# An RWKV attention in doubling blocks: r kept packed, its spread form copied by ScalarE

## The chip, the cores and the metric

One core of one Trainium2 chip. The time is the device time of one launch in microseconds; what is compared is the median of several runs. The engines are TensorE (PE in the profile; PEld is its weight load), VectorE (DVE), ScalarE (ACT), GpSimd (POOL) and SyncE (SP), which here only issues transfers.

## What is computed

Three stages in fp32: a recurrent attention with a decaying state per batch and head (4 batches, 8 heads, 768 tokens, 48 channels a head), a gated layer with RMS norm (384 to 1536 to 384), and a layer that takes the largest of three products (384 to 768 to 384).

```python
for t in range(S):
    kt, vt, rt, wt = (k[:, :, t], v[:, :, t], r[:, :, t], w[:, :, t])
    cur = np.einsum('bhd,bhe->bhde', u[None] * kt, vt)
    y[:, :, t] = np.einsum('bhd,bhde->bhe', rt, state + cur)
    state = wt[:, :, :, None] * state + np.einsum('bhd,bhe->bhde', kt, vt)
...
xn = x / rms * rms_g; g = xn @ w_gate
x1 = (silu(g) * (xn @ w_val)) @ w_out
...
out = maximum(maximum(x1 @ w1, x1 @ w2), x1 @ w3) @ w_out2
```

## The kernel before

The tokens are cut into six tiles of 128. In a tile the attention runs two batches ("a duo", j = 0 and 1) at a time. Channels lie on the partitions, two heads side by side: rows 0 to 63 hold the even head of a pair, rows 64 to 127 the odd one, and four pairs lie along the free axis. The recurrence is solved by doubling: at level L, blocks of h = 2^L tokens are joined in pairs. There are seven levels, 0 to 6. At each level and for each j:

- TensorE (`scores`, L477, levels 1 to 6) multiplies k with the right halves of r. Its moving operand needs r *spread*: `rB[j]` has a plane for the even heads, zero in the odd heads' rows, and one for the odd heads, zero in the others, so that one product of 128 rows yields the scores of each head by itself. Eight matmul records stand for one group of four matmuls.
- VectorE (`rescale_r_even`, L877) multiplies the right halves of r by the decay of the left block, in the even heads' rows, 64 rows of 256 columns; GpSimd (`rescale`, L1119 and L1124) multiplies the left halves of k (128 rows) and then the odd heads' r (64 rows). Both work on rB in place; at the last level they write to the packed `rD[j]`, whose left halves ScalarE copies from rB (`copy_r_left`, L682).
- VectorE takes the scores into A under a mask (`take_scores`, L900; a plain copy, L906, at level 6) and multiplies the block decays together (`double_blocks`, L887), which waits for r and k of the step.

After level 6, TensorE brings k back to tokens first (L511), computes the attended values from rD and the state (L495), and updates the state (L518).

**Slots.** Each engine has the same program of 18 slots a duo: slot 2L + j follows step j of level L, and four more come at the end (`TAIL_AT` = 14). A slot holds a part of the gated layer of the tile before: of each three parts, one is the gate product (TensorE L459 to L461, then ScalarE's sigmoid L672), one the value product (then VectorE's two products L853 and L856), one the output product (ScalarE's high part h_hi L676, GpSimd's low part h_lo L1091). Each engine goes through its own list strictly in this order.

**Tile 0** is different. In its first duo there is no gated layer yet; slots 3, 5, 7, 9, 11, 13 and 14 hold the splitting of one weight piece each: ScalarE writes the high part (`weight_piece`, L661), then VectorE the low part (L841, L843). In its second duo (`second_duo_slot`) a slot holds two parts of the layer, on half of the tokens (the batches of the first duo), and in slots 0 to 10 a weight piece behind them. ScalarE issues a piece's load two pieces ahead. Tile 1 also has half-sized parts (the other batches), without weights; from tile 2 on (a loop, `Fori`) the parts have full size. After the last tile come the last parts and the third stage, with three loops of its own.

**Queues.** SyncE issues the loads of k and w (`load_kw`), the tokens, r (`load_r`, two transfers of 128 KB, one per head row half) and v in the order written. At the start it waits until VectorE has zeroed rB before it loads r. ScalarE's queue issues the weight loads.

Of the kernel before, what the change touches and what calls it, by code (L numbers as in the profile page):

```python
# [45 lines left out]
def rwkv_moe_kernel(nc, rc, kc, wc, r, k, v, u, g_w1, v_w1, o_w1, rms_g, w1, w2, w3, o_w2, out):  # L46
# [17 lines left out]
    with ExitStack() as ctx:  # L64
# [34 lines left out]
        rD = [at_(f"rD{j}", [P, PAIRS, T]) for j in range(2)]  # L99
# [71 lines left out]
        r_even_scaled = sem("r_even_scaled")  # L171
        r_odd_scaled = sem("r_odd_scaled")
        r_left_copied = sem("r_left_copied")
# [65 lines left out]

        def r_rights(j, level, o):  # L240

            rows, h = HEAD_ROWS[o], 1 << level
            old = half(rB[j][rows, o, :, :], h, 1)
            return (half(rD[j][rows, :, :], h, 1) if level == LEVELS - 1 else old), old
# [94 lines left out]
        def _(sp):  # L339
# [114 lines left out]
        def _(pe):  # L454
# [8 lines left out]
            def scores(a, duo, level, j):  # L463
# [4 lines left out]
                after(pe, r_even_scaled, a, STEPS, n - 1)  # L468
                after(pe, r_odd_scaled, a, STEPS, n - 1)
# [10 lines left out]
            def attended(a, duo, j):  # L480
# [8 lines left out]
                after(pe, r_even_scaled, a, STEPS, n + 1)  # L489
                after(pe, r_odd_scaled, a, STEPS, n + 1)  # L490
                after(pe, r_left_copied, a, 2 * B, 2 * b + 2)
                after(pe, scores_used, a, SCORES, score(duo, LEVELS - 1, j) + 1)
                after(pe, v_in[j], a, 16 * DUOS, 16 * (duo + 1))
                for q in range(PAIRS):
                    mm(ps_desk[:, q * 2 * D:(q + 1) * 2 * D], rD[j][:, q, :], state[:, b * PAIRS + q, :],  # L495
                       start=(q == 0), stop=False)
# [150 lines left out]
        def _(act):  # L647
# [183 lines left out]
        def _(dve):  # L831
# [33 lines left out]
            def rescale_r_even(a, duo, level, j):  # L865

                n = step(duo, level, j)
# [358 lines left out]
```

## Time and profile before

| | |
|---|---|
| time, median of 3 runs | 1063.11 us (1062.24 to 1064.55) |
| span of the profiled execution | 1055.6 us |
| TensorE | 1010.7 us busy, 96% of the span |
| VectorE | 630.4 us, 60% |
| GpSimd | 493.3 us, 47% |
| ScalarE | 251.6 us, 24% |
| L1119 k product on GpSimd | 168 times, 142.9 us |
| L1124 odd r product on GpSimd, into rB | 144 times, 120.0 us (and 24 times into rD) |
| L877 even r product on VectorE, into rB | 144 times, 96.5 us (and 24 times into rD) |

The span is what the profiler sees from the first to the last instruction; the time of a run holds a little more around it. A busy share is an average over stages with different limits: what a change is worth has to be read in the stage where it acts, by looking at which engine's wait ends last there.

### The profile page before, as it was taken

Reading aid. Unit: us, or ns where it says so; the run is one execution under the profiler, and the core shown is the slowest. Engines: PE = TensorE matmul, PEld = TensorE weight load, DVE = VectorE, ACT = ScalarE, POOL = GpSimd, SP = SyncE. Lnnn points to the kernel's source line nnn. Section 1 sums busy time; section 2 is a strip of 40 time slices with the busy share of each in tenths; the row PEclk is TensorE's granted clock in tenths of the full one; section 3 lists DMA queues with packets and bytes.
Section 4 is the critical chain, followed back from the end, with each engine's and each line's share of the span. In section 5 each row is a group of like instructions: output and inputs, shape, how many; then the busy total and the mean of one; then the engine's idle time right before and its main releaser. Section 6 shows DMA issues by size and latency. Waiting matters only on the chain.

```text
span 1055.6 us, 17238 instructions
## 1 busy us (share of the span) xinstructions
PE 1010.7 (96%) x5760; PEld 884.7 (84%) x5760; DVE 630.4 (60%) x1083; ACT 251.6 (24%) x500; POOL 493.3 (47%) x548
## 2 busy tenths in 40 slices
PE   4778989899999999999999999999999999999998
PEld 4678988888888888888888888888788888888887
DVE  8978798987776877687787777444331312121221
ACT  1233312222122121312122212323331212121211
POOL 7655586767574756565756757121020201011111
PEclk9789999999999999999999999999999999999999
DMA  6533212303111221204030310211301010101000
GB/s 198 161 94 105 77 54 68 93 30 117 34 65 57 85 65 43 76 1 137 11 108 12 117 33 4 90 45 47 118 1 60 1 60 9 51 15 45 22 7 30
DMA packets 36216, 64.56 MB, mean 61 GB/s; under 512 B 4928, under 2 KB 22720, under 8 KB 36160
## 3 DMA queue, kind: packets, MB, share of 16 engines
q1 hardware_dynamic: 30288, 52.12, 15.4%
q10 hardware_dynamic: 5872, 11.80, 3.8%
q8 instruction: 23, 0.38, 0.1%
q14 instruction: 33, 0.27, 0.1%
HBM read 54.46 MB, written 9.44 MB: 61 GB/s over the span
## 4 chain that ended last, share of the span: by engine, by line
PE 84%; DVE 6%; POOL 5%; issue 3%; ACT 1%; DMA 0%; SPq 0%; POOLq 0%; DVEq 0%
PE ps_sc L477 9%; PE ps_acc L459 8%; PE ps_acc L461 8%; PE ps_acc L460 8%; PE ps_gate L459 6%; PE ps_val L459 5%; PE ps_val L461 5%; PE ps_gate L460 5%; PE ps_gate L461 5%; PE ps_val L460 5%; PE ps_desk L500 4%; PE ps_sc L460 2%; PE ps_sc L459 2%; PE ps_sc L461 2%; POOL kT L1119 2%
## 5 line engine op out<-in xcount | busy, mean ns | idle before, releaser
L477 PE MATMUL ps_sc<-rB,kT 128*128 128x128 f32 x1152 | 161.5, 287 | 25.8 <-DVE A L900 12.4
L477 PEld LDWEIGHTS ps_sc<-rB,kT 128*128 128x128 f32 x1152 | 154.9, 200 | 37.2 <-DVE rB L877 19.6
L1119 POOL TENSOR_TENSOR kT<-kT,wT 128x256 f32<-128x256 f32 x168 | 142.9, 851 | 86.0 <-PE ps_sc L477 58.1
L1184 POOL TENSOR_TENSOR h_lo<-h2f,h_hi 128x512 fp32r<-128x512 f32 x36 | 46.4, 1290 | 253.6 <-ACT h_hi L822 253.6
L1091 POOL TENSOR_TENSOR h_lo<-act_h,h_hi 128x512 fp32r<-128x512 f32 (+1 forms) x83 | 98.1, 1182 | 109.5 <-ACT h_hi L676 104.4
L1124 POOL TENSOR_TENSOR rB<-rB,wT 64x256 f32<-64x256 f32 x144 | 120.0, 833 | 11.3
L877 DVE TENSOR_TENSOR rB<-rB,wT 64x256 f32<-64x256 f32 x144 | 96.5, 675 | 37.8 <-PE ps_sc L477 28.4
L459 PE MATMUL ps_gate<-x_hi,wg_hi 128*128 128x512 f32 (+1 forms) x252 | 97.4, 386 | 7.7 <-DVE act_h L853 5.8
L676 ACT ACTIVATE h_hi<-act_h 128x512 fp32r<-128x512 f32 (+1 forms) x84 | 48.0, 571 | 227.9 <-DVE act_h L856 227.6
L900 DVE COPY_PREDICATED A<-mask,ps_sc 128x512 f32<-128x512 uint8 x120 | 98.7, 822 | 0.0
L672 ACT ACTIVATE act_h<-ps_gate 128x512 f32<-128x512 f32 (+1 forms) x84 | 45.0, 536 | 217.7 <-PE ps_gate L461 217.6
L459 PE MATMUL ps_val<-x_hi,wv_hi 128*128 128x512 f32 (+1 forms) x252 | 96.6, 383 | 0.0
L459 PE MATMUL ps_acc<-h_hi,wo_hi 128*128 128x512 f32 (+1 forms) x252 | 95.8, 380 | 0.5 <-POOL h_lo L1091 0.3
L461 PE MATMUL ps_val<-x_hi,wv_lo 128*128 128x512 f32 (+1 forms) x252 | 92.0, 365 | 0.0
L460 PE MATMUL ps_val<-x_lo,wv_hi 128*128 128x512 f32 (+1 forms) x252 | 91.8, 364 | 0.0
L460 PE MATMUL ps_gate<-x_lo,wg_hi 128*128 128x512 f32 (+1 forms) x252 | 91.5, 363 | 0.0
L461 PE MATMUL ps_gate<-x_hi,wg_lo 128*128 128x512 f32 (+1 forms) x252 | 91.4, 363 | 0.0
L461 PE MATMUL ps_acc<-h_hi,wo_lo 128*128 128x512 f32 (+1 forms) x252 | 90.9, 361 | 0.0
L460 PE MATMUL ps_acc<-h_lo,wo_hi 128*128 128x512 f32 (+1 forms) x252 | 90.8, 360 | 0.0
L1067 DVE TENSOR_TENSOR h2f<-h2f,ps_val 128x512 f32<-128x512 f32 x18 | 12.4, 688 | 108.1 <-PE ps_val L461 108.1
L887 DVE TENSOR_TENSOR wT<-wT 128x256 f32<-128x256 f32 (+6 forms) x168 | 65.1, 399 | 17.6 <-POOL rB L1124 16.1
L856 DVE TENSOR_TENSOR act_h<-act_h,ps_val 128x512 f32<-128x512 f32 (+1 forms) x84 | 51.4, 612 | 40.1 <-PE ps_val L461 38.9
(135 smaller groups left out, 2071.8 us busy)
## 6 DMA issues: line engine op xcount, KB each, us to landing
kT<-in_k_channels SPq DMA_DIRECT2D x24, 256.0 KB, 3.5
wT<-in_w_channels SPq DMA_DIRECT2D x24, 256.0 KB, 4.0
rB<-in_r_channels SPq DMA_DIRECT2D x48, 128.0 KB, 2.7
kL<-in_k_tokens SPq DMA_DIRECT2D x24, 192.0 KB, 2.4
rL<-in_r_tokens SPq DMA_DIRECT2D x24, 192.0 KB, 2.5
vL<-in_v_tokens SPq DMA_DIRECT2D x24, 192.0 KB, 2.4
x_scratch<-x1s SPq DMA_DIRECT2D x6, 768.0 KB, 4.3
xn<-x_scratch SPq DMA_DIRECT2D x6, 768.0 KB, 4.3
```

The costliest lines, as they stand in the source:

```text
L459: mm(dst, lhs[0], rhs[0], start=start, stop=False)
L460: mm(dst, lhs[0], rhs[1], start=False, stop=False)
L461: return mm(dst, lhs[1], rhs[0], start=False, stop=stop)
L477: last = mm(ps_sc[:, j, q * T:(q + 1) * T], kT[2 * duo + j][:, q, :], rights, start=True, stop=True)
L676: nc.scalar.activation(h_hi[:, f % 2, toks], act_h[:, f % 2, toks], ACT.Copy).then_inc(h_hi_done, 1)
L856: tt(hidden, hidden, ps_val[:, toks], ALU.mult).then_inc(val_used, 1)
L877: tt(new, old, block_decay(2 * duo + j, 1 << level, 0, HEAD_ROWS[0]), ALU.mult).then_inc(r_even_scaled, 1)
L887: tt(left, left, half(w[:, :, :], h, 1)[:, :, 0:1], ALU.mult).then_inc(tot_done, 1)
L900: nc.vector.copy_predicated(dst, every_head.broadcast_to([P, H, n, h]), src.rearrange("p (g n h) -> p g n h", g=H, h=h)).then_inc(scores_u ...
L1091: tt(h_lo[:, f % 2, toks], act_h[:, f % 2, toks], h_hi[:, f % 2, toks].bitcast(F32), ALU.subtract).then_inc(h_lo_done, 1)
L1119: tt(half(kT[b][:, :, :], h, 0), half(kT[b][:, :, :], h, 0), block_decay(b, h, 1), ALU.mult).then_inc(k_scaled, 1)
L1124: tt(new, old, block_decay(b, h, 0, HEAD_ROWS[1]), ALU.mult).then_inc(r_odd_scaled, 1)
```

## The change

r is loaded, scaled and used in the packed form `rP[j]` (rows as in k). One product on VectorE per level and j scales all 128 rows. GpSimd only scales k. ScalarE copies the right halves for the next level into rB, two copies of 64 rows (`spread_r`), and no longer copies left halves. The copies of level L + 1 stand in ScalarE's list at step j of level L, ahead of the slot, and wait for VectorE's product of that step. TensorE's scores wait for the copies. `load_r` becomes one transfer without a wait; the wait for the zeroed rB moves to ScalarE's first copy.

```diff
             def load_r(b, a):
-                for o, rows in enumerate(HEAD_ROWS):
-                    sp.dma_start(rB[b % 2][rows, o, :, :], rc[b, a, o]).then_inc(r_in[b % 2], 16)
+                sp.dma_start(rP[b % 2][:, :, :], rc[b, a].rearrange("o d q t -> (o d) q t")).then_inc(r_in[b % 2], 16)
...
                 load_kw(b, 0)
-                if b == 0:
-                    sp.wait_ge(rb_zeroed, 2)
                 load_r(b, 0)
...
             def scores(a, duo, level, j):
-                after(pe, r_even_scaled, a, STEPS, n - 1)
-                after(pe, r_odd_scaled, a, STEPS, n - 1)
+                after(pe, r_spread, a, 2 * SCORES, 2 * score(duo, level, j) + 2)
                 after(pe, k_scaled, a, STEPS, n - 1)
...
             def attended(a, duo, j):
-                after(pe, r_even_scaled, a, STEPS, n + 1)
-                after(pe, r_odd_scaled, a, STEPS, n + 1)
-                after(pe, r_left_copied, a, 2 * B, 2 * b + 2)
+                after(pe, r_scaled, a, STEPS, n + 1)
...
-            def copy_r_left(a, duo, j):
-                after(act, scores_done, a, SCORES, score(duo, LEVELS - 1, j) + 1)
-                for o, rows in enumerate(HEAD_ROWS):
-                    nc.scalar.activation(rD[j][rows, :, 0:T // 2], rB[j][rows, o, :, 0:T // 2], ACT.Copy
-                                         ).then_inc(r_left_copied, 1)
+            def spread_r(a, duo, level, j):
+                h = 1 << level
+                if isinstance(a, int) and a == duo == 0 and level == 1:
+                    act.wait_ge(rb_zeroed, j + 1)
+                after(act, scores_done, a, SCORES, score(duo, level, j) - 1)
+                after(act, r_scaled, a, STEPS, step(duo, level - 1, j) + 1)
+                for o, rows in enumerate(HEAD_ROWS):
+                    nc.scalar.activation(half(rB[j][rows, o, :, :], h, 1), half(rP[j][rows, :, :], h, 1), ACT.Copy
+                                         ).then_inc(r_spread, 1)
...
                     for j in range(2):
-                        if level == LEVELS - 1:
-                            copy_r_left(a, duo, j)
+                        if level < LEVELS - 1:
+                            spread_r(a, duo, level + 1, j)
                         slot(2 * level + j)
...
-            def rescale_r_even(a, duo, level, j):
+            def rescale_r(a, duo, level, j):
+                n, h = step(duo, level, j), 1 << level
                 if level:
                     after(dve, tot_done, a, STEPS, n - 1)
-                    after(dve, r_even_scaled, a, STEPS, n - 1)
+                    after(dve, r_scaled, a, STEPS, n - 1)
+                    after(dve, r_spread, a, 2 * SCORES, 2 * score(duo, level, j) + 2)
+                    after(dve, scores_done, a, SCORES, score(duo, level, j) + 1)
...
-                new, old = r_rights(j, level, 0)
-                tt(new, old, block_decay(2 * duo + j, 1 << level, 0, HEAD_ROWS[0]), ALU.mult).then_inc(r_even_scaled, 1)
+                rights = half(rP[j][:, :, :], h, 1)
+                tt(rights, rights, block_decay(2 * duo + j, h, 0), ALU.mult).then_inc(r_scaled, 1)
...
             def double_blocks(a, duo, level, j):
-                after(dve, r_even_scaled, a, STEPS, n + 1)
-                after(dve, r_odd_scaled, a, STEPS, n + 1)
+                after(dve, r_scaled, a, STEPS, n + 1)
                 after(dve, k_scaled, a, STEPS, n + 1)
...
-            def rescale(a, duo, level, j):
+            def rescale_k(a, duo, level, j):
-                after(pool, k_scaled, a, STEPS, n + 1)
-                new, old = r_rights(j, level, 1)
-                tt(new, old, block_decay(b, h, 0, HEAD_ROWS[1]), ALU.mult).then_inc(r_odd_scaled, 1)
-                after(pool, r_odd_scaled, a, STEPS, n + 1)
```

## Rows read from the trace of the kernel before

**Rows 1.** Busy time by stretch: start:end, length, PE, PEld, DVE, ACT, POOL, clock, DMA

```profile
0.00:50.00 50.00, 29.25 (x152) 26.71 (x152) 42.92 (x67) 11.50 (x18) 36.24 (x54) 0.86 0.60 182
50.00:106.00 56.00, 44.98 (x333) 42.91 (x333) 46.36 (x79) 17.39 (x35) 31.16 (x33) 0.91 0.34 100
106.00:217.00 111.00, 101.77 (x860) 98.64 (x859) 96.94 (x189) 28.23 (x75) 77.99 (x97) 1.00 0.24 74
220.00:664.00 444.00, 444.00 (x2622) 387.20 (x2620) 337.94 (x606) 100.80 (x205) 282.98 (x314) 1.00 0.18 57
```

**Rows 2.** What TensorE waited for, 50 to 106 us, then 106 to 217: us, times, longest

```profile
PE ps_gate L459 <- DVE act_h L853: 5.8, 6, 1.8
...
PE ps_sc L477 <- DVE A L900: 5.3, 4, 1.8
```

**Rows 3.** What VectorE waited for, 0 to 50 us, then 106 to 217

```profile
DVE wT L887 <- POOL rB L1124: 1.7, 1, 1.7
...
DVE wT L887 <- POOL rB L1124: 3.3, 5, 1.1
```

**Rows 4.** Two lines over the whole span: ns min/median/max, first and last start

```profile
L877 DVE TENSOR_TENSOR rB<-rB,wT x144: 406/452/1430, 7.9 to 648.4; 64x256 f32<-64x256 f32 x144
...
L682 ACT ACTIVATE rD<-rB x48: 402/417/421, 38.3 to 654.0; 64x256 f32<-64x256 f32 x48
```

**Rows 5.** VectorE by line and shape from 7, 50, 106 and 217 us: busy, mean ns

```profile
L877 DVE TENSOR_TENSOR rB<-rB,wT 64x256 f32<-64x256 f32 x12 | 7.4, 613 | 1.5 <-DMA rB<-in_r_channels 1.3 <-PE ps_sc L477 0.2
...
L877 DVE TENSOR_TENSOR rB<-rB,wT 64x256 f32<-64x256 f32 x12 | 9.3, 777 | 0.0
L887 DVE TENSOR_TENSOR wT<-wT 128x32 f32<-128x32 f32 x2 | 0.9, 430 | 0.0
...
L877 DVE TENSOR_TENSOR rB<-rB,wT 64x256 f32<-64x256 f32 x24 | 16.6, 697 | 0.1
...
L887 DVE TENSOR_TENSOR wT<-wT 128x32 f32<-128x32 f32 x16 | 3.3, 205 | 0.0
```

**Rows 6.** GpSimd's L1124 from 50 to 106 us, grouped; then two in order of time

```profile
L1124 POOL TENSOR_TENSOR rB<-rB,wT 64x256 f32<-64x256 f32 x12 | 12.3, 1025 | 0.9
...
69.90 1.65 DVE L843 SCALAR_TENSOR_TENSOR wg_lo<-x1s,gcol,wg_hi 128x768 fp32r<-128x768 f32 x1 [1.32 <-ACT wg_hi L661]
...
70.82 1.45 POOL L1124 TENSOR_TENSOR rB<-rB,wT 64x256 f32<-64x256 f32 x1
```

**Rows 7.** ScalarE, then VectorE, in order of time, 74.7 to 78 us

```profile
74.71 0.42 ACT L676 ACTIVATE h_hi<-act_h 128x256 fp32r<-128x256 f32 x1 [3.75 <-DVE act_h L856]
75.61 0.38 ACT L672 ACTIVATE act_h<-ps_gate 128x256 f32<-128x256 f32 x1 [0.48 <-PE ps_gate L461]
...
75.89 0.93 ACT L661 ACTIVATE wg_hi<-xn,gcol 128x768 fp32r<-128x768 f32 x1
...
76.41 0.96 DVE L877 TENSOR_TENSOR rB<-rB,wT 64x256 f32<-64x256 f32 x1
77.31 0.71 DVE L900 COPY_PREDICATED A<-mask,ps_sc 128x512 f32<-128x512 uint8 x1
77.92 1.52 DVE L843 SCALAR_TENSOR_TENSOR wg_lo<-xn,gcol,wg_hi 128x768 fp32r<-128x768 f32 x1
```

**Rows 8.** VectorE, then ScalarE, where the second half of tile 0 begins

```profile
55.77 0.42 DVE L877 TENSOR_TENSOR rB<-rB,wT 64x256 f32<-64x256 f32 x1
...
55.89 0.38 ACT L706 ACTIVATE x_hi<-ps_gate 128x256 fp32r<-128x256 f32 x1 [2.43 <-PE ps_gate L533]
```

**Rows 9.** ScalarE, then VectorE, at the start

```profile
12.00 0.20 ACT L775 ACTIVATE warm<-gcol 128x1 f32<-128x1 f32 x1 [1.00 <-DMA ub<-in_u]
...
13.63 1.06 DVE L877 TENSOR_TENSOR rB<-rB,wT 64x256 f32<-64x256 f32 x1
```

**Rows 10.** ScalarE, then TensorE, after the loop's top

```profile
335.16 0.60 ACT L672 ACTIVATE act_h<-ps_gate 128x512 f32<-128x512 f32 x1 [0.61 <-PE ps_gate L461]
...
336.99 1.98 PE L477 MATMUL ps_sc<-rB,kT 128*128 128x128 f32 x16
```

More of the change, by code:

```diff
@@ L98, in rwkv_moe_kernel @@
         rB = [at_(f"rB{j}", [P, 2, PAIRS, T]) for j in range(2)]
-        rD = [at_(f"rD{j}", [P, PAIRS, T]) for j in range(2)]
+        rP = [at_(f"rP{j}", [P, PAIRS, T]) for j in range(2)]
         kT = [at_(f"kT{b}", [P, PAIRS, T]) for b in range(B)]
@@ L170, in rwkv_moe_kernel @@
         u_taken = sem("u_taken")
-        r_even_scaled = sem("r_even_scaled")
-        r_odd_scaled = sem("r_odd_scaled")
-        r_left_copied = sem("r_left_copied")
+        r_scaled = sem("r_scaled")
+        r_spread = sem("r_spread")
         k_scaled = sem("k_scaled")
@@ L238, in block_decay @@
             return c.broadcast_to([rows.stop - rows.start, PAIRS * T // (2 * h), h])
[L240 to L244, printed above, removed]
         MASKED = LEVELS - 2
@@ L863, in last_hidden_lo @@
                    ).then_inc(last_h_lo, 1)
-            def rescale_r_even(a, duo, level, j):
-                n = step(duo, level, j)
+            def rescale_r(a, duo, level, j):
+                n, h = step(duo, level, j), 1 << level
                 if level:
                     after(dve, tot_done, a, STEPS, n - 1)
-                    after(dve, r_even_scaled, a, STEPS, n - 1)
+                    after(dve, r_scaled, a, STEPS, n - 1)
+                    after(dve, r_spread, a, 2 * SCORES, 2 * score(duo, level, j) + 2)
+                    after(dve, scores_done, a, SCORES, score(duo, level, j) + 1)
                 else:
                     after(dve, kw_in[2 * duo + j], a, 32, 32)
-                    after(dve, r_in[j], a, 32 * DUOS, 32 * (duo + 1))
-                if level:
-                    after(dve, scores_done, a, SCORES, score(duo, level, j) + 1)
-                new, old = r_rights(j, level, 0)
-                tt(new, old, block_decay(2 * duo + j, 1 << level, 0, HEAD_ROWS[0]), ALU.mult).then_inc(r_even_scaled, 1)
+                    after(dve, r_in[j], a, 16 * DUOS, 16 * (duo + 1))
+                rights = half(rP[j][:, :, :], h, 1)
+                tt(rights, rights, block_decay(2 * duo + j, h, 0), ALU.mult).then_inc(r_scaled, 1)
             def double_blocks(a, duo, level, j):
                 n, h = step(duo, level, j), 1 << level
-                after(dve, r_even_scaled, a, STEPS, n + 1)
-                after(dve, r_odd_scaled, a, STEPS, n + 1)
+                after(dve, r_scaled, a, STEPS, n + 1)
                 after(dve, k_scaled, a, STEPS, n + 1)
@@ L997, in duo_steps @@
                 for level in range(LEVELS):
-                    rescale_r_even(a, duo, level, 0)
+                    rescale_r(a, duo, level, 0)
                     take_scores(a, duo, level, 0)
                     slot(2 * level)
-                    rescale_r_even(a, duo, level, 1)
+                    rescale_r(a, duo, level, 1)
                     take_scores(a, duo, level, 1)
@@ L1111, in rescale @@
                     after(pool, tot_done, a, STEPS, n - 1)
-                    after(pool, r_odd_scaled, a, STEPS, n - 1)
                     after(pool, k_scaled, a, STEPS, n - 1)
+                    after(pool, scores_done, a, SCORES, score(duo, level, j) + 1)
                 else:
                     after(pool, kw_in[b], a, 32, 32)
-                    after(pool, r_in[j], a, 32 * DUOS, 32 * (duo + 1))
-                if level:
-                    after(pool, scores_done, a, SCORES, score(duo, level, j) + 1)
-                tt(half(kT[b][:, :, :], h, 0), half(kT[b][:, :, :], h, 0), block_decay(b, h, 1), ALU.mult
-                   ).then_inc(k_scaled, 1)
-                after(pool, k_scaled, a, STEPS, n + 1)
-                new, old = r_rights(j, level, 1)
-                tt(new, old, block_decay(b, h, 0, HEAD_ROWS[1]), ALU.mult).then_inc(r_odd_scaled, 1)
-                after(pool, r_odd_scaled, a, STEPS, n + 1)
+                lefts = half(kT[b][:, :, :], h, 0)
+                tt(lefts, lefts, block_decay(b, h, 1), ALU.mult).then_inc(k_scaled, 1)
             def inverse_rms(a, duo, j):
@@ L1135, in duo_steps @@
                     for j in range(2):
-                        rescale(a, duo, level, j)
+                        rescale_k(a, duo, level, j)
                         slot(2 * level + j)
```

2 lines of the change are left out of this document (1 added, 1 removed).

## The prediction

> **What bounds the kernel now.** I read the busy time by stretch first. From 220 to 664 us TensorE is busy for 444.00 of 444 us at full clock, so nothing done to the other engines can shorten that part, as long as they don't become late [rows 1]. In the first 217 us it idles: 20.8 us up to 50, 11.0 us from 50 to 106, 9.2 us from 106 to 217. Everything after 664 us is code that the change doesn't touch. So the whole case lies in tile 0 (up to about 106 us) and in the attention of tile 1 (up to 217 us).
>
> Next, who makes TensorE wait there. It is VectorE: its gate product L853 for 5.8 us, then its taking of scores L900 for 5.3 us [rows 2]. VectorE itself hardly idles (46.4 us busy of 56, 96.9 of 111 [rows 1]) and loses time on GpSimd in two ways. It waits outright for the odd heads' r, 1.7 and 3.3 us [rows 3]. And its operations stretch when a GpSimd operation runs beside them: the r product needs 0.406 us undisturbed [rows 4] but 0.613, 0.777 and 0.697 us on average in the three stretches; the small wT product of level 3 takes 0.430 us there against 0.205 us later [rows 5]. An L843 of 1.65 us lies across an L1124 of 1.45 us: each is held up by the other [rows 6].
>
> **The change, part by part.** The sum goes by differences; the profiled span is 1055.6 us, 7.5 us under the median of 1063.11 us, and I keep these 7.5 us. A difference of 0.2%, 2.1 us, is about what a measurement of this kernel can tell from none.
>
> *VectorE's r product* covers 128 rows instead of 64. The wT product of the same 256 columns on 128 rows runs at the same rate, so I cost this at nothing; the bound from the other side is none either, since the count stays 168.
>
> *GpSimd loses 168 products.* In 50 to 106 us they are 12.3 of its 31.2 us, 39% [rows 1, 6]. What VectorE gets back there: L877 loses 12 x (0.777 - 0.406) = 4.5 us, L887 about 12 x (0.430 - 0.205) = 2.7 us (one level's excess taken for all), and I add 1 us for the weight operations, so 8 us, of which 39% is 3.1 us. One more us for k's products, which meet a VectorE that now idles more. Before 50 us: 12 x (0.613 - 0.406) = 2.5, 14 x 0.225 = 3.1, another 0.5, so 6 us; 39% is 2.4 us, with the 1.7 us of plain waiting 4.1 us. From 106 to 217: 24 x (0.697 - 0.406) = 7.0 and 28 x 0.225 = 6.3 us, so 13 us; its 28 products are a smaller part of GpSimd's 78.0 us, and I take 30%: 3.9 us, with the 3.3 us of waiting 7.2 us.
>
> That two operations stretch rather than share is what the Trainium skill says too (SBUF — State Buffer, section "SBUF: two separate sides"): the port pair of VectorE and GpSimd is an exclusive lock, and the loser blocks for the whole instruction. By it a removed GpSimd operation may free more than its share of time, since each block moves the next one; that is rival A.
>
> *ScalarE gets 288 copies of 64x256 and loses 48.* The copies that it has take 0.417 us [rows 4], so 240 x 0.417 = 100 us on an engine with 251.6 us of work in 1055.6. Its load costs nothing; its order does. The two copies stand ahead of each slot's other work and wait for VectorE's product of the same step, so all that ScalarE had done early now comes after it. Who waits for that:
>
> - In tile 0's second half VectorE's low-part operation of each slot needs ScalarE's high part. In the slots with h_hi and the next sigmoid (1, 4, 7, 10), ScalarE does h_hi, sigmoid and high part from 74.71 to 76.8 us, before VectorE begins the step at 76.41; VectorE finds them done [rows 7]. Now they follow the r product: 0.83 + 0.42 + 0.28 + 0.93 = 2.46 us, of which VectorE's taking of scores covers 0.61 (77.31 to 77.92). New wait 1.85 us, three times, and 2.0 us in slot 1, which takes no scores: 7.5 us. In two slots with sigmoid first, VectorE's gate product waits 1.21 - 0.7 = 0.5 us: 1.0 us. In the slots where h_hi waits for VectorE anyway, nothing.
> - At this half's start ScalarE's x_hi at 55.89 falls behind copies that wait for the product of 55.77 + 0.42 [rows 8]: 56.19 + 0.83 = 57.0, so 1.1 us.
> - In the first half the high part follows the copies: 0.83 + 0.93 = 1.76 us, of which 0.8 is covered. 0.95 us at four levels, 0.4 at level 1, whose taking of scores is longer: 4.2 us. For new meetings with k's product I add 0.4 us.
> - At the start the first copy waits until ScalarE is through with its constants at 12.2 us [rows 9]. SyncE now issues r in one transfer, without waiting for the zeroing of rB, and reaches u's transfer nearly 3 us sooner, so I expect the copy at 10 to 12.2 us and the second r product of VectorE (13.63 us) between 13.1 and 15 us. Taken as 0; bounds -0.5 and +1.6.
> - In the tiles from 2 on the copies lie in slack, since a score group comes 5 us after the product that feeds it. The tightest place is the loop's top: ScalarE's sigmoid at 335.16, scores at 336.99 in two groups of 0.9 us [rows 10]. Copies at 335.2 to 336.0 and, after the sigmoid, 336.6 to 337.45 are 0.4 us early for the second group at 337.9. So 0; if the copy at level 1, with runs of two elements, takes twice 0.417, it is 1 us late at each of the four tops: bounds 0 and +4.
>
> *The wait that replaces the odd heads' one* on TensorE, for the copies instead of two scalings, is met 0.9 us after VectorE's product, where the taking of scores that it already waits for ends after 0.7 us. In tile 1 that lies within the slack of some 1.4 us per group.
>
> *Tile 1's attention* (106 to 217) has no weight pieces, so only relief: 7.2 us for VectorE against 9.2 us of TensorE idle. What is late next is TensorE itself, and the two levels where VectorE works on the neighbour terms (some 0.8 us left per half, and 0.9 us at the end). I take 6.5 us; bounds 4 and 9.
>
> *Sum.* First half of tile 0: -4.1 + 4.2 + 0.4 + 0 = +0.5. Second half: -4.1 + 7.5 + 1.0 + 1.1 = +5.5. Tile 1: -6.5. Later: 0. Together -0.5 us: 1055.1 us of span, 1062.6 us of time. That is no change.
>
> **The rivals.** A, the lock gives back more: all of VectorE's excess in tile 0 goes (14 us instead of the 6.5 us counted), as far as products can be freed of it. Then -7.5 more, less some 2 us where TensorE becomes the bound: -6, 1057 us. For it: blocks chain in rows 6. Against it: k's product starts on the same signal as r's and stays. Chance 0.34.
>
> B, slower: ScalarE's order in tile 0. Place: the weight slots; price: 1.85 us at three or four slots and 0.95 at five, which also thin TensorE's work, and its clock averages 0.86 and 0.91 there already [rows 1]. It decides from the point where tile 0 loses more than tile 1's 6.5 us and the 2.1 us of a visible change, 8.6 us. If the relief in tile 0 comes to half (4 us instead of 8.2), tile 0 loses 10 us, and with 1 to 3 us of low clock the sum is +5 to +7: 1069 us. Chance 0.22.
>
> C, the late copy at the loop's tops, +4 on top of the forecast: 1066 us. Chance 0.06. That the change does not do what it says cannot be: the products leave GpSimd's program.
>
> **How the numbers follow.** The forecast's case, the two effects cancelling within 2.1 us, has 0.38. Faster by over 0.2% is A and a fringe: 0.36. Slower is B and C: 0.28. Same: 0.36. The range takes in A's 1057 and B's 1069: 1056.5 to 1069.
>
> **What would show it.** Right: VectorE's L877 successor near 0.45 us on average and no wait of VectorE for GpSimd's r; new waits of VectorE for ScalarE's weight operation, 1.8 us each, in slots 1, 4, 7, 10 and 1 us at levels 1 to 5; tile 1's TensorE idle down to 2 or 3 us; no idle after 220 us. Wrong: weight waits absent (then A), TensorE idle in tile 1 still over 5 us (then B), idle at each loop top (C).

## The result, and the profile after

The changed kernel takes 1071.3 us (1069.93 to 1072.36) against 1062.67 us of the kernel before beside it: 1.0085 times, 95% interval 1.0062 to 1.0107. Executed again, beside other executions of the kernel before, it took 1068.7 us, 1.0059 times (1.0042 to 1.0076). It is slower by 6 to 9 us; the forecast was 0.5 us faster, with 1069.0 as the upper end.

First the page's engine line and the granted clock in 40 slices of the changed kernel, then its busy time by stretch (start:end, length, PE, PEld, DVE, ACT, POOL, clock, DMA share, GB/s).

```profile
PE 1016.3 (95%) x5760; PEld 889.0 (83%) x5760; DVE 619.7 (58%) x1083; ACT 351.4 (33%) x740; POOL 348.5 (33%) x380
...
PEclk9679999999999999999999999999999999999999
```

```profile
0.00:50.00 50.00, 24.45 (x124) 22.25 (x124) 36.36 (x61) 18.82 (x35) 21.40 (x39) 0.79 0.54 177
50.00:106.00 56.00, 44.38 (x302) 42.20 (x302) 34.56 (x65) 22.42 (x49) 12.93 (x18) 0.83 0.26 77
106.00:217.00 111.00, 101.49 (x843) 98.38 (x843) 96.18 (x194) 45.96 (x115) 52.79 (x65) 0.98 0.27 80
```

The work moved as planned: GpSimd went from 493 to 349 us busy, ScalarE from 252 to 351. Against [rows 1] VectorE is busy for 12 us less between 50 and 106 us, and TensorE still gets less done there (302 matmuls, not 333), at a lower clock. Half of the 12 us is work that now lies behind 106 us: for the same work, between the first two marks of the next table, VectorE is busy for 53.7 us where before's second trace has 59.7.

To see where time goes I take four marks in TensorE's program: its first transposition of x (L520; L533 before) in tile 0's second half, at the start and at the end of tile 1's attention, and the last one, at the end of tile 5. In the trace of before they stand at 55.2, 126.7, 215.1 and 671.9 us. So the second half of tile 0 lasts to 126.7 us on TensorE; the prediction ended it at 106, with its last scores, but TensorE waits for nothing between 106 and 126.7 in before, so no wait changes its term by that. The table gives how much later each kernel reaches the marks; "in tile 1" and "in the tops" are what the third and the fourth mark add to the one ahead. "Low" is the time at the lower clock level (granted clock 0.5) in the first 120 us or so.

| kernel (short name) | low | 55.2 | 126.7 | 215.1 | 671.9 | in tile 1 | in the tops |
|---|---|---|---|---|---|---|---|
| before, first trace | 24 | 0 | 0 | 0 | 0 | 0 | 0 |
| before, second trace (e12) | 41 | +6.3 | +7.0 | +6.9 | +6.9 | -0.1 | 0 |
| changed | 44 | +6.1 | +11.7 | +8.6 | +10.6 | -3.1 | +2.0 |
| changed, second trace (e11) | 44 | +6.0 | +11.7 | +8.6 | +10.9 | -3.1 | +2.3 |

The second line decides how the others are read. The same kernel before, executed again, reaches the first mark 6.3 us later, because TensorE's clock was low for longer. Here is the stretch 35 to 70 us of before, of before again and of the changed kernel; the last three numbers are clock, DMA share and GB/s.

```profile
35.00:70.00 35.00, 26.42 (x171) 25.05 (x172) 27.75 (x52) 11.34 (x25) 17.11 (x20) 0.76 0.46 135
```

```profile
35.00:70.00 35.00, 27.39 (x131) 25.98 (x131) 25.54 (x46) 9.24 (x22) 16.40 (x18) 0.57 0.41 131
```

```profile
35.00:70.00 35.00, 26.23 (x120) 24.93 (x121) 21.55 (x43) 10.00 (x22) 7.85 (x9) 0.51 0.42 133
```

TensorE is busy for 26 to 27 us in all three, but gets through 171 matmuls in one and 120 to 131 in the others. So the first trace of before was an unusually quick execution (span 1055.6), and the changed kernel has to be compared with the second one (span 1062.5, time 1064.26). Then the stages read: first half of tile 0 -0.2 us (+6.1 against +6.3), second half +5.0, tile 1 -3.1, the rest up to the last mark +2.0. Together +3.7 us at the last mark (+4.0 with e11), and 5.4 to 8.0 us in the times of the two pairs of executions.

The rest of the 5.4 to 8.0 us lies behind the last mark, in code that the change doesn't touch: 383.8 us in before's three traces (e4 is the third), 388.1 and 385.2 us in the changed kernel's, 383.7 to 388.2 us in the other runs. There ScalarE issues three loads of weights for the third stage. They take its queue 0.46, 0.45 and 0.45 us in before, 1.74, 1.00 and 1.72 us in the changed kernel's first trace, and TensorE then waits 2.6 us for the gate product behind them (1.2 us in e11, not at all in before). e7 below has these waits (1.3 us) without a single copy of the change, and e3 has the copies and no such wait; what makes the issues long is open.

**Second half of tile 0.** What TensorE waits for, 60 to 122 us in the changed kernel, then 60 to 118 us in before's second trace (us in total, times, longest):

```profile
PE ps_gate L449 <- DVE act_h L844: 6.3, 6, 1.5
PE ps_acc L449 <- POOL h_lo L1081: 5.2, 4, 2.5
PE ps_gate L449 <- ACT x_hi L697: 2.1, 1, 2.1
PE ps_gate L520 <- DVE xn L971: 1.5, 1, 1.5
```

```profile
PE ps_gate L459 <- DVE act_h L853: 6.3, 6, 1.8
PE ps_gate L533 <- DVE xn L981: 1.5, 1, 1.5
PE ps_sc L477 <- DVE A L900: 1.1, 1, 1.1
PE ps_gate L459 <- ACT x_hi L706: 1.0, 1, 1.0
```

x_hi is 1.1 us later, as forecast. TensorE's waits for VectorE's gate product are no shorter, for all that VectorE meets less of GpSimd; VectorE's own waits for ScalarE's high parts have grown by 7.6 us (3.9 to 11.5), just what was forecast for them. And a wait has come that before does not have: GpSimd's low part h_lo, 5.2 us. The slot of a high part in the changed kernel (ScalarE, then VectorE, then GpSimd):

```profile
84.61 0.42 ACT L673 ACTIVATE rB<-rP 64x256 f32<-64x256 f32 x1 [1.78 <-PE ps_sc L466]
84.87 0.34 ACTq L640 DMA_DIRECT2D x1s<-in_moe_w_val  x1
85.06 0.41 ACT L673 ACTIVATE rB<-rP 64x256 f32<-64x256 f32 x1
85.50 0.42 ACT L663 ACTIVATE h_hi<-act_h 128x256 fp32r<-128x256 f32 x1
85.82 0.37 ACT L659 ACTIVATE act_h<-ps_gate 128x256 f32<-128x256 f32 x1
86.09 0.92 ACT L648 ACTIVATE wg_hi<-xn,gcol 128x768 fp32r<-128x768 f32 x1
```

```profile
84.10 0.42 DVE L868 TENSOR_TENSOR rP<-rP,wT 128x256 f32<-128x256 f32 x1
84.44 0.70 DVE L890 COPY_PREDICATED A<-mask,ps_sc 128x512 f32<-128x512 uint8 x1
87.04 1.18 DVE L834 SCALAR_TENSOR_TENSOR wg_lo<-xn,gcol,wg_hi 128x768 fp32r<-128x768 f32 x1 [1.91 <-ACT wg_hi L648]
```

```profile
85.99 0.73 POOL L1081 TENSOR_TENSOR h_lo<-act_h,h_hi 128x256 fp32r<-128x256 f32 x1 [3.22 <-ACT h_hi L663]
```

ScalarE idles 1.78 us until r is scaled (the profile names the scores, which VectorE's product at 84.10 waits for too, so they were done), then does copy, copy, h_hi, sigmoid and high part in a row, and VectorE waits 1.91 us. h_hi, which depends on nothing of this step (its input was ready at 82.78), comes at 85.50, GpSimd's low part at 85.99, and TensorE's output product at 86.77, after a wait of 1.14 us. All four waits for h_lo (0.78, 1.14, 0.83 and 2.47 us) come in such slots, 1, 4, 7 and 10, where h_hi follows the copies at once. [rows 7] show h_hi, sigmoid and high part before: done by 76.8 us, before VectorE asks.

**Tile 1.** The start of level 5, all engines but TensorE's weight work left out:

```profile
161.85 0.94 POOL L1107 TENSOR_TENSOR kT<-kT,wT 128x256 f32<-128x256 f32 x1 [1.29 <-PE ps_sc L466]
162.22 0.85 DVE L868 TENSOR_TENSOR rP<-rP,wT 128x256 f32<-128x256 f32 x1
...
163.17 0.85 ACT L673 ACTIVATE rB<-rP 64x256 f32<-64x256 f32 x2 [3.46 <-DVE rP L868]
...
164.08 1.16 PE L466 MATMUL ps_sc<-rB,kT 128*128 128x128 f32 x8 [1.33 <-ACT rB L673]
```

The r product takes 0.85 us, beside k's product; the two copies start when it ends; TensorE has waited 1.33 us for them. Before, this gap was 1.76 us, for the taking of scores:

```profile
152.99 1.13 PE L477 MATMUL ps_sc<-rB,kT 128*128 128x128 f32 x8 [1.76 <-DVE A L900]
```

Of tile 1's 28 r products 11 take over 0.6 us. Nine of them lie across a product of k and end 0.28 us after it, and two lie across GpSimd's product of r and k.

**Loop tops.** ScalarE and TensorE in the changed kernel, where the loop starts anew (rows of other operations left out):

```profile
344.61 0.91 ACT L673 ACTIVATE rB<-rP 64x256 f32<-64x256 f32 x2 [1.43 <-DVE rP L868]
...
345.54 0.60 ACT L659 ACTIVATE act_h<-ps_gate 128x512 f32<-128x512 f32 x1
...
346.16 0.89 ACT L673 ACTIVATE rB<-rP 64x256 f32<-64x256 f32 x2
...
347.29 1.15 PE L466 MATMUL ps_sc<-rB,kT 128*128 128x128 f32 x8 [0.37 <-ACT rB L673]
```

This is rival C's picture; in [rows 10] the scores follow the sigmoid without a gap.

### The profile page after: what moved, and what is told of

Same layout as the page of the kernel before. It is cut to its first block, busy times and chain, and to the rows that moved or that the text cites. A ratio compares the mean times of both kernels' runs of the same rounds, so it can differ in the third digit from the quotient of the medians.

```text
span 1070.5 us, 17381 instructions
## 1 busy us (share of the span) xinstructions
PE 1016.3 (95%) x5760; PEld 889.0 (83%) x5760; DVE 619.7 (58%) x1083; ACT 351.4 (33%) x740; POOL 348.5 (33%) x380
## 4 chain that ended last, share of the span: by engine, by line
PE 85%; DVE 4%; issue 4%; ACT 3%; POOL 1%; ACTq 1%; DMA 0%; DVEq 0%; SPq 0%; POOLq 0%
PE ps_sc L466 10%; PE ps_acc L449 8%; PE ps_acc L451 8%; PE ps_acc L450 8%; PE ps_gate L449 6%; PE ps_gate L451 5%; PE ps_gate L450 5%; PE ps_val L449 5%; PE ps_val L451 5%; PE ps_val L450 5%; PE ps_desk L487 4%; PE ps_sc L450 2%; PE ps_sc L449 2%; PE ps_sc L451 2%; PE ps_desk L482 2%
## 5 line engine op out<-in xcount | busy, mean ns | idle before, releaser
L673 ACT ACTIVATE rB<-rP 64x256 f32<-64x256 f32 x288 | 121.0, 420 | 193.9 <-DVE rP L868 186.3
L466 PEld LDWEIGHTS ps_sc<-rB,kT 128*128 128x128 f32 x1152 | 152.7, 198 | 37.7 <-ACT rB L673 27.3
L1081 POOL TENSOR_TENSOR h_lo<-act_h,h_hi 128x512 fp32r<-128x512 f32 (+1 forms) x83 | 94.5, 1138 | 197.7 <-ACT h_hi L663 197.7
L868 DVE TENSOR_TENSOR rP<-rP,wT 128x256 f32<-128x256 f32 x168 | 107.6, 645 | 57.2 <-PE ps_sc L466 47.6
L844 DVE TENSOR_TENSOR act_h<-act_h,ps_gate 128x512 f32<-128x512 f32 (+1 forms) x84 | 50.5, 602 | 45.4 <-ACT act_h L659 45.1
L1057 DVE TENSOR_TENSOR h2f<-h2f,ps_val 128x512 f32<-128x512 f32 x18 | 12.4, 687 | 108.1 <-PE ps_val L451 108.1
```

The costliest lines, as they stand in the source:

```text
L466: last = mm(ps_sc[:, j, q * T:(q + 1) * T], kT[2 * duo + j][:, q, :], rights, start=True, stop=True)
L673: nc.scalar.activation(half(rB[j][rows, o, :, :], h, 1), half(rP[j][rows, :, :], h, 1), ACT.Copy).then_inc(r_spread, 1)
L844: tt(hidden, hidden, ps_gate[:, toks], ALU.mult).then_inc(gate_used, 1)
L868: tt(rights, rights, block_decay(2 * duo + j, h, 0), ALU.mult).then_inc(r_scaled, 1)
L1081: tt(h_lo[:, f % 2, toks], act_h[:, f % 2, toks], h_hi[:, f % 2, toks].bitcast(F32), ALU.subtract).then_inc(h_lo_done, 1)
```

## The experiments

Each time stands beside executions of the kernel before on the same chip; the factor and its 95% interval are against these.

**The order on ScalarE in tile 0 (e1, e2).** e1 puts ScalarE's slot ahead of the copies in tile 0, except in the second half's slots 2, 5, 8, ..., which hold a high part of h that waits for VectorE's product of the same step; e2 does so in the first half alone.

```diff
                     for j in range(2):
+                        i = 2 * level + j
+                        behind = isinstance(a, int) and a == 0 and (duo == 0 or i % 3 != 2)
+                        if behind:
+                            slot(i)
                         if level < LEVELS - 1:
                             spread_r(a, duo, level + 1, j)
-                        slot(2 * level + j)
+                        if not behind:
+                            slot(i)
```

> The changed kernel, but in tile 0 ScalarE does a slot's work (weight high part, sigmoid, h_hi) ahead of the copies of r, except in the slots of the second half where h_hi has to wait for VectorE anyway (2, 5, 8, ...). If ScalarE's order in tile 0 is what costs, VectorE's waits for weight high parts go (5 times 1.2 us in the first half, 4 times 1.9 us in the second), and the time falls from the changed kernel's 1071 us by 9 to 12 us to about 1061. If the order costs only little and the low clock of TensorE between 35 and 69 us is a matter of its own, it falls by 3 us or less.

> The changed kernel, with ScalarE's slot put ahead of the copies only in the first half of tile 0 (the high parts of the weight pieces); the second half keeps the changed kernel's order. Both halves together gave 1054.8, 16.5 us under the changed kernel. By my terms the first half had 4.2 us of weight waits and the second 8.5 us of weight and gate waits. If the terms add up: 1071.3 - 4.5 = 1067 us. If the low clock that followed in the first half (0.5 of full speed from 35 to 69 us) is set off by those waits, more: 1062 to 1064 us.

e1: 1054.8 us (1051.5 to 1057.2), 0.9925 of before (0.990 to 0.9951), more than was expected of it. e2: 1063.5 us, 1.0022 (1.0002 to 1.0042), as expected if the low clock comes with these waits; its ten executions have a median mean granted clock of 0.985, the changed kernel's eight 0.979.

| kernel | low | 55.2 | 126.7 | 215.1 | 671.9 | in tile 1 | in the tops |
|---|---|---|---|---|---|---|---|
| e1 | 37 | +2.2 | -0.7 | -3.8 | -2.0 | -3.1 | +1.8 |
| e2 | 24 | -2.8 | +2.9 | -0.2 | +1.7 | -3.1 | +1.9 |

Against the changed kernel's 1068.7 to 1071.3 us the order in tile 0 is worth 14 to 16 us; by the marks 12.4 us of it lie in tile 0 (+11.7 to -0.7), and tile 1 and the tops are unchanged. Some of this is the clock, which was up for longer in e1. In executions of like mean granted clock it is 13 us (1056.5 and 1057.2 us at 0.982 against 1069.9 at 0.981), and e2's first-half order alone 2 to 5 us of it. In e1's second half TensorE waits 4.6 us for the gate product instead of 6.3 and not at all for h_lo:

```profile
PE ps_gate L449 <- DVE act_h L849: 4.6, 7, 1.1
PE ps_gate L520 <- DVE xn L976: 1.5, 1, 1.5
PE ps_gate L449 <- ACT x_hi L697: 1.0, 1, 1.0
PE ps_sc L466 <- ACT rB L673: 0.6, 1, 0.6
```

e1 and e2 are identical in the first half, yet differ there by 5.0 us, with 37 and 24 us of low clock: a single trace cannot price an edit in the first half.

**The clock (e3, e4, e11, e12).** e3 is the changed kernel and e4 the kernel before, each with products of the identity matrix added on TensorE in the first half of tile 0, so that its clock stays up.

```diff
-            run_tile_0(duo_steps, nothing, x_transposed, part, end)
+            def keep_warm(count):
+                for _ in range(count):
+                    mm(ps_gate[:, 0:T], ident[:, :], ident[:, :], start=True, stop=True)
+
+            pe.wait_ge(mask_step, 2 * MASKED + 2)
+            keep_warm(24)
+            run_tile_0(duo_steps, lambda i: keep_warm(8 if i > 1 else 0), x_transposed, part, end)
```

> The changed kernel with extra TensorE products of the identity into an unused bank: 24 before the first scores, 8 in each slot of tile 0's first half from slot 2 on (they compute nothing that is used). If the low granted clock from 35 to 69 us is what took 4 us in the attended values of the first half and 1 us at the start of the second, the transposes at 61.3 us come at 57 us and the time falls by 4 to 6 us to about 1066. If the clock is only an accompaniment of ScalarE's order, it stays within 1.5 us of 1071.

> The kernel before with the same extra products. It had a low clock from 34.7 to 44.9, 55.2 to 62.0 and 75.7 to 79.1 us. If the clock costs in tile 0, it becomes 2 to 5 us faster than 1062.7. If VectorE alone sets the pace there, no difference.

e3: 1065.9 us (1065.2 to 1066.95), e4: 1058.95 us (1058.63 to 1061.04), against 1061.2 of before. The granted clock from 35 to 70 us is 1.00 in both (e3, then e4):

```profile
35.00:70.00 35.00, 31.72 (x276) 30.82 (x274) 25.57 (x50) 11.03 (x25) 10.57 (x12) 1.00 0.45 142
```

```profile
35.00:70.00 35.00, 33.24 (x292) 32.76 (x290) 28.44 (x53) 9.64 (x22) 20.37 (x22) 1.00 0.48 147
```

Difference at full clock: 6.95 us; by the marks of e3 against those of e4, tile 0 +8.3 (+9.6 against +1.3), tile 1 -3.1, tops +2.1, and nothing behind the last mark. The slowdown is there with the clock up, and e3's waits in the second half are those of the changed kernel (h_lo 5.3 us, gate product 6.1). The clock is not what makes the kernel slower. The second half, where no products are added, has +5.5 of the 8.3 us. The first half's +2.8 is less sure, since the added matmuls stand in TensorE's queue ahead of real ones. e3 came out at the expected time, but its first mark at 62.7 us and not at 57, which the added products may have held back.

> The changed kernel once more, on the chip of the kernels sent with it. The first half of tile 0 ran at half the granted clock from 35 to 69 us, and the tail after 690 us had 4.3 us more than before. If both belong to the change: 1071 us and the same two stretches. If they fall differently in each execution, as the tail's seems to: 1066 to 1070 us, with a low stretch of another length.

> The kernel before once more, for a second trace. Its first trace has 20 us of half clock in 27 to 62 us and a span 7.5 us under the median. If the clock stretch of the change is its own, this one shows again some 20 to 24 us of half clock in the first 110 us, against 37 to 44 in the changed kernel and its variants; if it is chance, any length from 20 to 45.

Their marks are in the first table. The low stretch of 34 us is in both traces of the changed kernel. But before's second trace has one almost as long. The 31 executions of before beside e5 ran from 1057.4 to 1065.1 us; the first profiled one (span 1055.6 and the 1.8 us around it) is at their lower end.

Whether the changed kernel draws a long low stretch more often can be read from the mean granted clock of every execution. The 74 executions of before beside the experiments have 0.980 to 0.990, median 0.984. The changed kernel's eight have 0.978, 0.978, 0.979, 0.979, 0.979, 0.981, 0.984 and 0.986. So it does, by about 0.005, which is some 10 us more at the lower level. Over before's executions the time rises by 0.25 us with each us of low clock (a straight line through the 74), so this is an estimated 2 to 3 us of the slowdown. At like clock the rest is left: at 0.979 to 0.981, 1069.6 to 1070.4 us against 1062.5 to 1065.1 (median 1064.1), and at 0.984 to 0.986, 1067.8 and 1067.9 us against 1060.0 to 1063.5 (median 1062.2): 6 us either way.

**Tile 1: what the relief is worth, and what takes it back (e7, e5, e9, e10).** e7 is the kernel before without GpSimd's product of the odd heads' r at levels 0 to 5 (it leaves out their decay). e5 is the changed kernel with k's product held until r's is done. e9 is the changed kernel with the scores reading rP, so that they don't wait for the copies (it leaves out the separation of the two heads). e10 is both, with k held at levels 0 to 5. e7, e9 and e10 thus compute something else and only show time.

```diff
             def rescale_k(a, duo, level, j):
...
+                after(pool, r_scaled, a, STEPS, n + 1)
                 lefts = half(kT[b][:, :, :], h, 0)
```

```diff
             def scores(a, duo, level, j):
-                after(pe, r_spread, a, 2 * SCORES, 2 * score(duo, level, j) + 2)
+                after(pe, r_scaled, a, STEPS, n - 1)
...
-                    rights = rB[j][:, :, q, :].rearrange("p o (n two h) -> p o n two h", two=2, h=h)[:, :, :, 1, :]
+                    both = rP[j][:, q:q + 1, :].broadcast_to([P, 2, T])
+                    rights = both.rearrange("p o (n two h) -> p o n two h", two=2, h=h)[:, :, :, 1, :]
```

> The kernel before without GpSimd's product on the odd heads' r at levels 0 to 5 (left out, so the scores of odd heads are not decayed) and without the waits for it: the relief of the change alone, with none of ScalarE's copies. By the sum of the prediction it is 4.1 + 4.1 + 6.5 us, so 1048 us. If the products on k, which start on the same signal as those on r, take over the meetings with VectorE, it is about half: 1055 us.

> The changed kernel (1071.3 us), with GpSimd's product of k held until VectorE's product of r of the same step is done. In the changed kernel both start on the same signal, and in tile 1's attention (106 to 217 us) VectorE's operations take 16.7 us longer than the shortest of their kind, where the kernel without GpSimd's r product had 13.2. Theory K (tile 1 gained only 3.1 us instead of 8.5 because the r product now meets the k product): the r product runs undisturbed at 0.41 us, the copies behind it are earlier by 0.2 to 0.3 us per step, tile 1 gains another 2 to 5 us, tile 0 1 to 2: 1065 us. Theory L (what is missing is the latency of the two copies, 0.9 us between VectorE's product and TensorE's scores): the collision only moves to the taking of scores, and nothing is gained, or k is late and up to 2 us are lost: 1070 to 1073 us.

> The changed kernel, but TensorE's scores read r from the packed rP for both heads of a pair and wait for VectorE's product alone; ScalarE's copies stay in their places and nobody on TensorE reads or waits for them. It leaves out the separation of the two heads, so the scores are the sums of both. Theory L (latency of the copies holds TensorE in tile 1): tile 1's relief goes from 3.1 to about 8 us, the gaps of 1.33 us at the scores disappear, and tile 0 gains another 1 to 2 us: 1063 to 1065 us, the rest over the kernel before being the order in tile 0. Theory K (collisions of the r product with the k product): tile 1 as in the changed kernel within 1 us: 1070 us.

> The changed kernel with both parts of what could hold tile 1: scores read r from rP and don't wait for the copies (this leaves out the separation of the two heads), and GpSimd's k product is held behind the r product at levels 0 to 5. Alone the first gave 0.7 us of tile 1, the second 2.2 us. If these two mechanisms are all that separates the changed kernel (3.1 us gained in tile 1) from the kernel without GpSimd's r product (8.5 us), both together give 7.5 to 8.5 us there. If they only add: 6 us, and 2.5 us have another cause.

| kernel | time | low | 126.7 | in tile 1 | in the tops |
|---|---|---|---|---|---|
| e7 | 1047.2 (0.9869, 0.9844 to 0.9893) | 27 | -3.0 | -8.5 | 0 |
| e5 | 1064.15 (1.0036, 1.0019 to 1.0054) | 44 | +8.2 | -5.3 | +2.0 |
| e9 | 1064.96 (1.0023, 1.0000 to 1.0045) | 44 | +9.3 | -3.8 | +0.3 |
| e10 | 1063.2 (1.0001, 0.9983 to 1.0019) | 41 | +6.7 | -5.4 | +1.1 |

What TensorE waited for in tile 1 and some us around it, in the changed kernel, e5, e10 and e7:

```profile
PE ps_sc L466 <- ACT rB L673: 2.7, 2, 1.3
PE ps_sc L498 <- DVE A L896: 2.5, 4, 1.0
```

```profile
PE ps_sc L498 <- POOL kT L1108: 3.8, 4, 1.5
...
PE ps_sc L466 <- ACT rB L673: 0.6, 3, 0.2
```

```profile
PE ps_sc L499 <- DVE A L897: 4.0, 4, 1.7
```

```profile
PE ps_sc L510 <- DVE A L906: 1.9, 4, 0.7
```

And VectorE's r product, in the changed kernel from 114 to 228 us and in e5 from 110 to 222, which takes in a few of tile 0 and tile 2 (instructions, busy us, mean ns):

```profile
L868 DVE TENSOR_TENSOR rP<-rP,wT 128x256 f32<-128x256 f32 x33 | 20.1, 617 | 1.6 <-PE ps_sc L466 1.6
```

```profile
L868 DVE TENSOR_TENSOR rP<-rP,wT 128x256 f32<-128x256 f32 x33 | 14.1, 435 | 2.6 <-PE ps_sc L466 2.6
```

Three readings. The relief itself was not overrated: e7 has 8.5 us of it in tile 1, more than my 6.5. The real change keeps only 3.1, and holding k's product back returns 2.2: r's product goes from 617 to 435 ns (638 to 439 in tile 1 alone) and the waits for copies from 2.7 to 0.6 us. The copies' own latency is worth 0.7 us in tile 1 by e9, where the wait passes to VectorE's taking of scores (3.0 us), and nothing more on top of e5 (e10). e9's time is the one that the latency theory gave, but its gain lies in tile 0 (2.4 us) and in the tops (1.7). Of the 3.1 us left between e10 and e7, 2.1 are waits at level 6. There e10 shows

```profile
160.04 1.02 POOL L1089 TENSOR_TENSOR prod<-rL,kL 128x384 f32<-128x384 f32 x1
160.15 1.32 DVE L903 TENSOR_TENSOR xn<-v_prev,diag_prev 128x384 f32<-128x384 f32 x1
```

where e7 has 0.60 us for the same VectorE operation. The changed kernel has 0.69 there, so it is holding k that brings this meeting about. In the tops e9 is at +0.3: without the copies 1.7 of the 2.0 us are gone, and that is shown. e10 is at +1.1 though nobody waits for a copy there; what k's hold adds in the tops is open.

**Can both be had? (c2, c3, e6, e13).** c2 is e1 and e5 together. c3 holds k only at levels 0 to 5 and from tile 1 on makes both level-1 copies ahead of ScalarE's first slot. e6 is the changed kernel with this last edit alone. e13 is c3 with k free at level 0 too and, from tile 1 on, GpSimd's product of r and k (L1088) one level earlier.

```diff
+                        early = duo == 0 and not (isinstance(a, int) and a == 0)
+                        if early and level == 0:
+                            if j == 0:
+                                spread_r(a, duo, 1, 0)
+                                spread_r(a, duo, 1, 1)
-                        if level < LEVELS - 1:
+                        elif level < LEVELS - 1:
```

```diff
-                    if level == LEVELS - 2:
+                    if level == (LEVELS - 2 if isinstance(a, int) and a == 0 else LEVELS - 3):
                         r_times_k(a, duo, 0)
```

> The kernel with ScalarE's slots ahead of the copies in tile 0 (1054.8 us), with GpSimd's product of k held until VectorE's product of r of the step is done. Theory K: tile 1 gains 2 to 5 us more: 1051 us. Theory L: no gain, 1054 to 1056 us.

> The changed kernel with three edits: ScalarE's slots ahead of the copies in tile 0; GpSimd's k product held behind the r product at levels 0 to 5 (with level 6 held too, TensorE then waited 3.8 us in tile 1 for k at L498, where it otherwise waits 2.5 us for VectorE's L896); both level-1 copies ahead of ScalarE's first slot from tile 1 on. The two first edits with level 6 held gave 1053.5. If the rise of 2.0 us over the three loop tops is ScalarE's second copy behind the sigmoid, it goes: -2.0, and -0.6 to -1.3 for level 6: 1050.5 us. If the loop tops' rise had another cause: 1052.5 us.

> The changed kernel (1068.7 to 1071.3 us) with one edit: from tile 1 on ScalarE makes both level-1 copies ahead of its first slot. If the rise at the loop tops (2.0 us over three) is the second copy behind the sigmoid: 2 us less, 1067 to 1069 us, no gap of TensorE at the tops. If the sigmoid, now behind four copies, makes VectorE's gate product late and with it the next scores: the gap moves on to the next scores and nothing is gained.

> The kernel c3 (slots ahead of copies in tile 0, k held behind r, both level-1 copies first), but k is held at levels 1 to 5 only, and from tile 1 on GpSimd's product of r and k stands one level earlier (after level 4). If its meeting with VectorE's neighbour term is what is left in tile 1: the L498 waits (1.6 us, twice) fall to 0.7 and tile 1 gains 1.5 to 2 us more than c3's 4.5. If it only meets other operations instead: no gain there. If holding k at level 0 took the place of the late copy at the loop tops, their 2.5 us fall to 0.5 or less. Both right: 1050 us; neither: 1053.5.

| kernel | time | low | 126.7 | in tile 1 | in the tops |
|---|---|---|---|---|---|
| c2 | 1053.5 (0.9939, 0.9916 to 0.9961) | 31 | -4.0 | -5.3 | +2.0 |
| c3 | 1053.7 (0.9924, 0.991 to 0.9938) | 17 | -7.5 | -4.5 | +2.5 |
| e6 | 1070.3 (1.008, 1.0052 to 1.0108) | 41 | +11.6 | -2.7 | +2.4 |
| e13 | 1057.2 (0.9932, 0.9906 to 0.9957) | 31 | -3.7 | +2.9 | +2.4 |

c2 and e1 cannot be told apart by their factors (0.9939 and 0.9925), so what k's hold gives by the marks (5.3 for 3.1 us in tile 1) does not show in the time once the order is right. The early copies gain nothing: in e6 the wait moves on. The sigmoid now follows four copies, VectorE's products follow it, and TensorE waits 0.8 us in all for the next taking of scores instead of 1.1 us for copies (230 to 660 us):

```profile
PE ps_sc L466 <- DVE A L895: 0.8, 3, 0.3
```

In e13 the waits at level 6 fell by 0.4 us in all (3.3 against c3's 3.7; the longest 1.2 against 1.6), and new ones of 0.9 us came for copies. Its profiled execution was also the slowest of six and had two stretches of 6.8 us at the lower clock inside tile 1, which none of the others has there, so its +2.9 in tile 1 says little. That the meeting of L1088 is what remains between e10 and e7 is thus read from rows, not shown by a run. c2, c3 and e1 are the best versions, 0.6 to 0.8% below before (1053.5, 1053.7 and 1054.8 us); their intervals overlap, and e1 has a single edit.

## Why the prediction was wrong

Two steps failed. The relief of tile 1 was put at -6.5 us and came to -3.1, because k's product took over the meetings that r's left (holding k back gives 2.2 us of it back, e5). And the copies at the loop tops were put in slack at nothing and cost 2.0 us of TensorE's time, 1.7 of them gone when the scores don't need the copies (e9). What ScalarE's order costs in tile 0 was in the sum; e1 shows that it is the largest cost of the change.

Measured is the first trace of the changed kernel against the second of before, which has the like clock; a second number is from the pair at full clock (e3 and e4).

- **First half of tile 0**: forecast +0.5, measured -0.2 and +2.8. The two pairs disagree, so whether this term was right is open. The waits for high parts are there: 0.56, 1.15, 1.22, 1.24 and 1.25 us, 5.4 in all against 4.2, and taking them away (e2) is worth 2 to 5 us at like clock.
- **Second half**: forecast +5.5, measured +5.0 and +5.5. The size was right, the path only in part, so it is partly luck that the sum fits so well. The waits of VectorE at slots 1, 4, 7 and 10 are 2.13, 1.91, 1.79 and 1.79 us (2.0 and 1.85 forecast), x_hi is 1.1 us late as forecast. But on TensorE the waits for the gate product are 6.3 us in both kernels, so the relief seems to pay for these, and what is new there is h_lo, 5.2 us. Its waits come in just the slots 1, 4, 7 and 10 that I priced with "New wait 1.85 us": there I followed the high part to VectorE and never h_hi to GpSimd and to TensorE. Both halves together were forecast at +6.0; the like pair has +4.8, the pair at full clock +8.3.
- **Tile 1**: forecast -6.5, bounds -4 to -9, measured -3.1 and -3.1. This is the term that failed beyond its bounds. "k's product starts on the same signal as r's and stays" stood in the text as an argument against rival A only. It means that r's product, now on the path through the copies to TensorE, still meets k's: 638 ns on average in tile 1, hardly less than before's 697 and far from the 406 of an undisturbed one. I took 30% of VectorE's excess, 3.9 us, as gone because GpSimd's r product is a part of its work. Counted over all of VectorE's operations between the marks of tile 1, each against the shortest of the same line and shape in its trace, the excess is 19.9 and 20.2 us in the traces of before, 17.7 and 17.8 in those of the changed kernel, 13.3 in e7 and 11.0 in e5. So 2.3 us went where e7 loses 6.7, and k's product took the other meetings over: held back, it gives up 6.7 us more.
- **Loop tops**: forecast 0, bounds 0 to +4, measured +2.0 to +2.3, and 0.3 without the copies' wait. The arithmetic of 0.4 us to spare let the copies begin at 335.2, the time of the sigmoid before; 8.6 us later that is 343.8. But they began at 344.61, since VectorE's product itself starts only at 344.15. Before, it starts at 334.67, which 8.6 us later is 343.3. At the three tops it starts 5.9 to 6.2 us after TensorE's transposition in both traces of the changed kernel and in e5 and e9, and 5.3 to 5.6 us in those of before and in e7; the profile names nothing that it waits for, so the cause of this part is open. Of the 2.0 us, 1.1 are plain waits (0.4 at each top); the rest is in score groups that read longer in these three tiles, 25.5, 25.4 and 25.4 us against 25.2.
- **The base**. I wrote that I keep the 7.5 us between span and median. Only 1.8 us of these are around the span (1072.26 against 1070.5, 1064.26 against 1062.5); the others were the clock of that one execution. It did no harm to the sum, which goes by differences, but [rows 1] showed me 0.86 and 0.91 as the kernel's own clock where other executions have less.

The terms' errors, -0.7, -0.5, +3.4 and +2.0 to 2.3, come to +4.2 to 4.5 us and bring the -0.5 to about +4. Two things lie between that and the medians' 6.5 to 8.6 us, and the sum had neither: the longer low stretch (2 to 3 us, estimated above), and the 1.4 and 4.4 us behind 671.9 us, where I wrote that the change touches nothing. Rivals B and C were both partly what happened, and I had them as alternatives and not as terms that can come together: C's 2 us on top of B's 1069 are 1071. Of the signs, that for B was right: TensorE idle in tile 1 of over 5 us (6.1 between the marks). So was C's, idle at the loop tops. Of the signs of being right, VectorE's waits in slots 1, 4, 7 and 10 came, but its r product averages 645 ns over the whole run and not 450.

Rival A drew on what the Trainium skill says of VectorE and GpSimd (SBUF — State Buffer, section "SBUF: two separate sides"). The rows agree with an exclusive lock: 0.85 us for r's product beside k's 0.94, 0.42 alone, and its end 0.28 us after k's in all nine such meetings of tile 1. (That is less than 0.42, so a part of its work seems to be done by the time k's product ends.) What they add is that its cost goes by which two operations start together, not by how much work GpSimd has: in tile 1 GpSimd's busy time fell from 65.7 to 42.3 us and VectorE's excess by 2.3 us only.

## What to carry to other kernels

When an operation is taken from a contended engine, ask which other operation starts on the same signal as the one that stays: if it does, the meeting isn't removed, it is handed on. An in-order engine with slack still sets times for all who read its results; whoever puts a waiting operation at the head of each of its steps must follow every result behind it to its last reader (here ScalarE's h_hi to GpSimd to TensorE), and putting the work that is ready first turned a loss of 0.6 to 0.9% into a gain of 0.75%. A profile is one execution: before pricing a stage where the clock moves, get a second one, and compare executions of like mean granted clock.

## What the runs showed of the hardware

Executions of one kernel on one chip differ by up to 7.7 us (1057.4 to 1065.1), and the time goes with TensorE's mean granted clock (0.25 us for each us at the lower level). Two traces differ in the first 110 us: 24 us at the lower level in one trace and 41 in another, the first mark 6.3 us apart. On another chip, where 17 executions ran from 1057.8 to 1063.7, the identity products that hold the clock at 1.00 from 35 to 70 us narrow this to 1058.6 to 1061.0 and bring the kernel before from 1061.2 to 1058.95 (0.9978, 0.9966 to 0.9991). A product of VectorE that lies across one of GpSimd ended 0.28 us after it, whether that made it 0.61 or 1.08 us long, where it takes 0.42 undisturbed. ScalarE's 64x256 copy of a strided half took 0.417 us at levels 2 to 6 and 0.438 at level 1, so the run length that I feared costs 0.02 us.
